# RWKV attention with two MLPs on one core: the first units rearranged

## Chip, core and metric

The kernel runs on one core of a Trainium2 chip. The metric is the device time of one execution, in microseconds (us). TensorE multiplies, VectorE (DVE), ScalarE (ACT) and GpSimd (POOL) do the rest, and SyncE (SP) issues the DMA transfers.

## What is computed

Everything is float32. Attention with a decaying state over 4 batches, 8 heads, 768 steps, head size 48; its output goes through two MLPs for 3072 tokens of width 384.

```python
state = zeros(B, H, D, D)                      # 4, 8, 48, 48
for t in range(768):
    cur = einsum('bhd,bhe->bhde', u[None] * k[t], v[t])
    y[t] = einsum('bhd,bhde->bhe', r[t], state + cur)
    state = w[t][..., None] * state + einsum('bhd,bhe->bhde', k[t], v[t])
x = y as [3072, 384]
h = x @ w_in                                   # 384 x 1024
solu = h * softmax(h)
x = layernorm(solu) * g_ln @ w_out             # 1024 x 384
g = relu(x @ w2_in) ** 2                       # 384 x 2048
out = g @ w2_out                               # 2048 x 384
```

## The kernel before

The 768 steps are cut into NU = 12 units of T = 64 steps. Within a unit the decay products are built by doubling: `w_products` makes six levels of products of w, and at each of the 6 levels `carry` (VectorE) multiplies halves of r and `carry_k` (GpSimd) halves of k by them, `right_halves` (ScalarE) copies r into a layout for TensorE, `level` (TensorE) multiplies k with r and `pair_scores` (VectorE) takes the wanted scores out of PSUM into `att`. `place` and `take_level5` (ScalarE) finish the scores. Each step is done for two halves (h = 0, 1) of the heads. At level 0 stands `level_bonus`: k with r of odd steps, and the product `uk` = k times u with r. That product is made on GpSimd (`products`), which also decays the state (`decay_state`) and clears the score tile.

Then come `k_natural` (transposes of k in TensorE, copied by `take_k` into the same buffer `uk`), `output` (state and scores times r and v; two copies `take_output` take it to `x_t`) and `state_step` with `add_state`. `repack` is six small DMA transfers that move heads into rows; `x_high` and `x_low` split x into two parts, since float32 products are made of three products of such parts.

PSUM has 8 banks: `flex` has four (banks 0 and 1 for attention, 2 and 3 for the first MLP), `hid` one and `acc` three for the second MLP. The first MLP runs one unit behind the attention: `hidden1` for two token tiles t of 128 tokens and two column halves f, `row_max`, `exps`, `gate`, `squares`, `variance`, `inverse_root`, `normalise`, then `ln_transpose` with `ln_high` and `ln_low`, and `narrow1` for three row tiles d with `take_narrow`. The second MLP works on blocks of two units, from turn 3 on: `up` into `hid`, `relu`, `square`, `down` into `acc`, sixteen times a block.

One turn handles one unit of attention. In each turn every engine has its own written order: the tables SP_AT, PE_AT, DVE_AT, ACT_AT and POOL_AT give each step a place in the queue of its engine (a number for each half, tile or piece). Turns 0, 1 and 2 have tables of their own, as have turns 3 and 4; from turn 5 on two tables alternate. Engines work their queue strictly in order and wait for each other with semaphores. Steps placed alongside the attention in turns 0 to 4 are the weights' pieces: 24 pieces are loaded (`load_piece`), and split by ScalarE (`piece_high`) and VectorE (`piece_low`); the second MLP's are also stored to DRAM (`keep_piece`) and reloaded later (`load_w2`).

Before the first turn SyncE issues, in this order, k, r_pair (two), u, w, r and gain of unit 0, then weight pieces and v. VectorE, ScalarE and GpSimd wait with `wait_ge(u_loaded, 32)` for both u and gain before any turn. In `state_step` TensorE waits for `x_ready` since it writes the banks from which the output is copied; the next `level_bonus` waits for `state_ready`, the end of the add, for the same reason; and `k_natural` waits for `att_ready`, since the transposes go over the last scores in banks 0 and 1. `output` waits for `knat_ready`. Half 0 of `hidden1` for t = 1 waits for `solu_ready`, as both token tiles use banks 2 and 3. ScalarE's activations all show line 888, its common helper.

## Time and profile before

| | us |
|---|---|
| median of 3 runs | 826.29 |
| lowest and highest | 823.72, 828.02 |
| the profiled execution | 825.71 |
| its span, first to last instruction | 824.1 |
| TensorE busy in the span | 768.9 |
| VectorE, ScalarE, GpSimd busy | 493.6, 416.5, 200.0 |

The mean granted TensorE clock is 0.992 of full speed. How to read the rows: a time at the left is the start from the span's beginning, in us, then the duration; `x32` is a count of merged instructions; `[2.22 <-DVE state L703]` says that the engine had been idle for 2.22 us before and that this instruction released it. PEld is the weight load of TensorE, PE the matmul. L511 is line 511 of the kernel.

### The profile page before, as it was taken

The numbers are of one execution on the slowest core, as the hardware profiler recorded it, in microseconds if no ns is written. First come the engines' busy times: TensorE is split into PE (matmuls) and PEld (weight loads), VectorE is DVE, ScalarE is ACT, GpSimd is POOL, SyncE is SP. The second block draws the span as 40 slices with busy tenths as digits, with TensorE's granted clock in tenths as the row PEclk, the third lists the DMA queues.
The fourth block names the chain that finished last, engine by engine and source line by source line (L and its number), as shares of the span: only waits on it lengthen the run. The fifth ranks groups of instructions, "written<-read, shape, count | busy, mean of one in ns | idle before, by whom it ended". The sixth has DMA issues, their size and how long they took to land.

```text
span 824.1 us, 25081 instructions
## 1 busy us (share of the span) xinstructions
PE 768.9 (93%) x10480; PEld 642.2 (78%) x10480; DVE 493.6 (60%) x985; ACT 416.5 (51%) x853; POOL 200.0 (24%) x277
## 2 busy tenths in 40 slices
PE   1567879999999999999999999999999999999997
PEld 1456768788788788788788788788789788888886
DVE  7787576867856745736754746853755763453333
ACT  3855474845744643644653644553654562333232
POOL 5453334212413301412400501510501210000000
PEclk9989999999999999999999999999999999999999
DMA  7423454174375344535455444344544232453652
GB/s 237 122 86 80 164 163 133 63 244 176 117 243 160 112 173 164 168 104 165 130 180 158 138 141 166 131 149 147 179 141 147 98 118 82 153 163 121 227 192 102
DMA packets 32272, 122.34 MB, mean 148 GB/s; under 512 B 4896, under 2 KB 10144, under 8 KB 32160
## 3 DMA queue, kind: packets, MB, share of 16 engines
q1 hardware_dynamic: 32160, 120.74, 44.3%
q8 instruction: 83, 1.36, 0.7%
q14 instruction: 29, 0.24, 0.1%
HBM read 102.24 MB, written 17.30 MB: 145 GB/s over the span
## 4 chain that ended last, share of the span: by engine, by line
PE 87%; DVE 4%; ACT 3%; issue 2%; DMA 2%; SPq 1%; POOL 0%; DVEq 0%; POOLq 0%; ACTq 0%
PE hid L558 24%; PE acc L571 24%; PE flex L511 13%; PE flex L542 11%; PE flex L449 4%; PE flex L525 2%; PE flex L475 2%; PE flex L464 1%; PE flex L482 1%; PE flex L493 1%; PE flex L435 1%; DVE r_t L689 1%; DMA gain<-in_gcol 1%; DVE w_up L675 1%; PE flex L430 1%
## 5 line engine op out<-in xcount | busy, mean ns | idle before, releaser
L558 PE MATMUL hid<-y_hi,w 128*128 128x512 f32 x576 | 198.0, 398 | 0.1
L571 PE MATMUL acc<-g_hi,w 128*128 128x512 f32 x576 | 195.7, 396 | 1.4 <-DVE g_lo L766 0.9
L888 ACT ACTIVATE r_right<-r_t 64x256 f32<-64x256 f32 x240 | 100.2, 417 | 69.2 <-DVE r_t L689 53.8
L762 DVE TENSOR_TENSOR act<-act 128x512 f32<-128x512 f32 x96 | 68.9, 718 | 105.0 <-ACT g_hi L888 105.0
L571 PEld LDWEIGHTS acc<-g_hi,w 128*128 128x128 f32 x576 | 108.1, 188 | 25.2 <-issue 1.2
L558 PEld LDWEIGHTS hid<-y_hi,w 128*128 128x128 f32 x576 | 108.1, 188 | 23.8 <-issue 0.5
L888 ACT ACTIVATE act<-hid 128x512 f32<-128x512 f32 x96 | 57.3, 597 | 118.5 <-PE hid L558 118.1
L1098 POOL TENSOR_TENSOR k_t<-k_t,w_up 128x256 f32<-128x256 f32 x120 | 86.0, 733 | 113.8 <-PE flex L449 85.0
L558 PE MATMUL hid<-y_lo,w 128*128 128x512 f32 x288 | 112.5, 391 | 0.0
L571 PE MATMUL acc<-g_lo,w 128*128 128x512 f32 x288 | 112.4, 390 | 0.0
L542 PE MATMUL flex<-ln_hi,out_hi 128*128 128x256 f32 x288 | 81.1, 282 | 1.6 <-issue 0.8
L542 PE MATMUL flex<-ln_hi,out_lo 128*128 128x256 f32 x288 | 80.8, 281 | 0.0
L542 PE MATMUL flex<-ln_lo,out_hi 128*128 128x256 f32 x288 | 80.8, 281 | 0.0
L766 DVE TENSOR_TENSOR g_lo<-act,g_hi 128x512 fp32r<-128x512 f32 x96 | 68.3, 712 | 3.3
L689 DVE TENSOR_TENSOR r_t<-r_t,w_up 128x256 f32<-128x256 f32 x120 | 66.3, 568 | 6.3 <-ACT r_right L888 5.7
L449 PEld LDWEIGHTS flex<-r_right,k_t 128*32 128x32 f32 x3072 | 34.6, 116 | 40.7 <-issue 28.6
L888 ACT ACTIVATE g_hi<-act 128x512 fp32r<-128x512 f32 x96 | 60.7, 632 | 6.1 <-PE acc L571 3.3
L449 PE MATMUL flex<-r_right,k_t 128*32 128x32 f32 x3072 | 41.2, 205 | 23.2 <-DVE att L665 13.7
L511 PE MATMUL flex<-in_hi,x_hi 128*128 128x512 f32 x144 | 61.2, 425 | 1.0 <-DVE x_lo L708 0.7
L571 PEld LDWEIGHTS acc<-g_lo,w 128*128 128x128 f32 x288 | 54.2, 188 | 10.0
L558 PEld LDWEIGHTS hid<-y_lo,w 128*128 128x128 f32 x288 | 54.2, 188 | 10.0
L511 PE MATMUL flex<-in_hi,x_lo 128*128 128x512 f32 x144 | 58.3, 405 | 0.0
(92 smaller groups left out, 1199.6 us busy)
## 6 DMA issues: line engine op xcount, KB each, us to landing
w<-split_w SPq DMA_DIRECT2D x80, 768.0 KB, 4.6
split_w<-w SPq DMA_DIRECT2D x16, 768.0 KB, 5.9
k_t<-in_kT SPq DMA_DIRECT2D x12, 512.0 KB, 3.9
r_pair<-in_rT SPq DMA_DIRECT2D x24, 256.0 KB, 4.3
w_t<-in_wT SPq DMA_DIRECT2D x12, 512.0 KB, 6.0
r_t<-in_rT SPq DMA_DIRECT2D x12, 512.0 KB, 6.5
v_n<-in_vN SPq DMA_DIRECT2D x12, 384.0 KB, 5.4
out<-o_stage SPq DMA_DIRECT2D x5, 768.0 KB, 7.3
```

The costliest lines, as they stand in the source:

```text
L449: last = mm(flex[block_rows(q % 2 * 2 + n), h, c:c + BK], k_t[:, o:o + BK], right[:, :, o // 2:(o + BK) // 2], start=True, stop=True)
L475: mm(flex[half_rows(i), b2, x * T:(x + 1) * T], state[u % 2][:, q, i], r_t[:, q * T:(q + 1) * T], start=x == 0, stop=False, skip_group_che ...
L511: last = mm(flex[:, MLP1 + f, :], x[:, k, toks], w[:, k, cols], start=n == 0, stop=n == len(terms) - 1)
L525: last = nc.tensor.transpose(flex[:, MLP1 + half, n * P:(n + 1) * P], solu[:, t, j * P:(j + 1) * P], ident[:, :])
L542: last = mm(flex[:, MLP1 + d % 2, 0:TOK], w[:, j, rows], x[:, j, :], start=n == 0, stop=n == len(terms) - 1)
L558: last = mm(hid[:, :], w2[:, j % RING, w, k * P:(k + 1) * P], y[:, k, :], start=n == 0, stop=n == len(terms) - 1)
L571: last = mm(acc[:, d], w2[:, j % RING, w, rows], gx[:, j % 2], start=j == 0 and n == 0, stop=j == J2 - 1 and n == 2, skip_group_check=True)
L689: e.tensor_tensor(right, right, left_w, ALU.mult).then_inc(r_ready, 1)
L762: e.tensor_tensor(act[:, j % 2], act[:, j % 2], act[:, j % 2], ALU.mult).then_inc(g_ready, 1)
L766: e.tensor_tensor(g_lo[:, j % 2], act[:, j % 2], g_hi[:, j % 2].bitcast(F32), ALU.subtract).then_inc(glo_ready, 1)
L888: return nc.scalar.activation(out_, in_, func, **more)
L1098: e.tensor_tensor(left, left, right_w, ALU.mult).then_inc(k_ready, 1)
```

## The change

- On the zero state of unit 0 nothing is done any more: no `decay_state` in turn 0; `add_state` of unit 0 copies instead of adding.
- `products` moves from GpSimd to ScalarE: for each half two activations of 128x256 with u as a scale per row.
- Unit 0 is loaded in halves with semaphores of their own (`r_first` and so on, `wait_loaded`); ScalarE issues the two halves of w, then u between them, then gain. gain has its own semaphore, awaited at the first piece of the output weights.
- In units 0, 1 and 2 (`FILL = 3`) the transposes of k and the state step go to banks of the second MLP, idle until then (`side_bank`: `hid` and the last of `acc`). There `k_natural` waits for the state of the unit before and not for the scores, `state_step` waits for the copies of k and not for the output's, and the next `level_bonus` waits for the output's copies and not for the state.
- In the first MLP's units 0 and 1 the second token tile goes to `acc[:, 0:2]` (`h_banks`), and its `hidden1` doesn't wait for the first tile's gate; nor do the transposes wait for it.
- `output` waits for `att_ready`, and for `knat_ready` only from unit 3 on.
- All tables of order are written anew. In turns 1 and 2 `hidden1` of the first token tile stands ahead of level 1, and in turn 1 the first half of the second tile between the halves of level 1; in turn 3 `hidden1` comes first. SyncE issues v ahead of the repack in turns 1, 3 and 4.

```diff
 SP_AT = [
-    {"load_w_pair": 1, "load_k": 3, "repack": 6, "load_r": 5, "load_v": 9, "load": {5: 0, 6: 2, 7: 4, 9: 7, 8: 8}},
-    {"load_w_pair": 1, "load_k": 0, "repack": 2, "load_r": 4, "load_v": 7, "keep": {9: 6, 8: 8}, "load": {11: 3, 10: 5}},
+    {"load_w_pair": 1, "load_k": 5, "repack": 6, "load_r": 4, "load_v": 8, "load": {5: 0, 7: 2, 6: 3, 8: 7, 9: 9}},
+    {"load_w_pair": 1, "load_k": 2, "repack": 4, "load_r": 5, "load_v": 3, "keep": {8: 6, 9: 8}, "load": {10: 0, 11: 7}},
...
 PE_AT = [
-    {"level": ((0, 1), (2, 3), (4, 5), (6, 7), (8, 9), (10, 11)), "k_natural": 12, "output": 13, "state": 14},
-    {"level": ((0, 1), (4, 5), (6, 7), (8, 10), (11, 12), (14, 15)), "k_natural": 16, "output": 18, "state": 20, "hidden1": ((2, 3), (9, 13)), "ln":
-     (17, 19), "narrow": (21, 22, 23)},
-    {"level": ((0, 1), (2, 5), (6, 7), (8, 9), (11, 12), (14, 15)), "k_natural": 16, "output": 18, "state": 20, "hidden1": ((3, 4), (10, 13)), "ln":
-     (17, 19), "narrow": (21, 22, 23)},
+    {"level": ((0, 1), (2, 3), (4, 5), (6, 7), (8, 9), (10, 11)), "k_natural": 12, "output": 13, "state": 14, "read_state": -1},
+    {"level": ((0, 1), (4, 6), (7, 8), (9, 10), (11, 13), (14, 16)), "k_natural": 17, "output": 18, "state": 20, "hidden1": ((2, 3), (5, 12)), "ln":
+     (15, 19), "narrow": (21, 22, 23)},
+    {"level": ((0, 1), (4, 5), (6, 7), (8, 9), (11, 12), (14, 15)), "k_natural": 17, "output": 18, "state": 20, "hidden1": ((2, 3), (10, 13)), "ln":
+     (16, 19), "narrow": (21, 22, 23)},
...
 ACT_AT = [
-    {"right": ((1, 4), (6, 8), (9, 10), (11, 13), (14, 17)), "place": (15, 16), "level5": (18, 19), "k_natural": 20, "output": 22, "x_high": 24,
-     "piece": {0: 0, 1: 2, 2: 3, 3: 5, 4: 7, 5: 12, 6: 21, 7: 23}},
+    {"products": (1, 2), "right": ((0, 3), (5, 7), (9, 11), (13, 14), (16, 18)), "place": (15, 17), "level5": (19, 20), "k_natural": 24, "output": 22,
+     "x_high": 26, "piece": {0: 4, 1: 6, 2: 8, 3: 10, 4: 12, 5: 21, 6: 23, 7: 25}},
+    {"products": (0, 2), "right": ((1, 3), (5, 6), (8, 9), (12, 13), (14, 16)), "place": (15, 17), "level5": (19, 20), "k_natural": 23, "output": 24,
+     "x_high": 27, "exp": (7, 18), "squares": (11, 21), "ln_high": (22, 25), "narrow": (26, 28, 29), "piece": {8: 4, 9: 10}},
...
+        def wait_loaded(eng, first, rest, u, h, each=16):
+
+            if u or h:
+                eng.wait_ge(rest, each * (u + 1))
+            else:
+                eng.wait_ge(first, each)
+
...
+        def side_bank(u, n):
+
+            if u >= FILL:
+                return flex[:, n]
+            return acc[:, KD - 1] if n else hid[:, :]
+
+        def h_banks(u, t):
+
+            return acc[:, 0:2] if t and u < FILL - 1 else flex[:, MLP1:MLP1 + 2]
...
-            load_k(0)
-            load_w_pair(0)
-            sp.dma_start(u_rows[:, :], uT).then_inc(u_loaded, 16)
-            sp.dma_start(w_t[:, :], wT[0]).then_inc(w_in, 16)
-            load_r(0)
-            sp.dma_start(gain[:, :], gcol).then_inc(u_loaded, 16)
+            for h in range(2):
+                sp.dma_start(k_t[:, half(h)], kT[0][:, half(h)]).then_inc(k_in if h else k_first, 16)
+                for i in range(2):
+                    sp.dma_start(r_pair[half_rows(i), i, half(h)], rT[0][half_rows(i), half(h)])                        .then_inc(rp_in if h else rp_first, 16)
+                sp.dma_start(r_t[:, half(h)], rT[0][:, half(h)]).then_inc(r_in if h else r_first, 16)
...
+                wait_loaded(pe, k_first, k_in, u, h)
+                wait_loaded(pe, rp_first, rp_in, u, h, 32)
                 if h == 0:
-                    pe.wait_ge(k_in, (u + 1) * 16)
-                    pe.wait_ge(rp_in, (u + 1) * 32)
-                    wait(pe, state_ready, u * 2)
+                    wait(pe, x_ready if u <= FILL else state_ready, u * 2)
...
                     pe.wait_ge(k_ready, half_count(u, LEVELS - 1, h))
-                    pe.wait_ge(att_ready, u * 2 + h + 1)
+                    if u < FILL:
+                        wait(pe, state_ready, u * 2)
+                    else:
+                        pe.wait_ge(att_ready, u * 2 + h + 1)
...
-                pe.wait_ge(knat_ready, (u + 1) * 2)
+                pe.wait_ge(att_ready, (u + 1) * 2)
+                if u >= FILL:
+                    pe.wait_ge(knat_ready, (u + 1) * 2)
...
-                pe.wait_ge(x_ready, u * 2 + 2)
+                if u < FILL:
+                    pe.wait_ge(knat_ready, u * 2 + 2)
+                else:
+                    pe.wait_ge(x_ready, u * 2 + 2)
...
-                elif f == 0:
+                elif f == 0 and u >= FILL - 1:
                     pe.wait_ge(solu_ready, u * 2 + 1)
...
-            v.wait_ge(u_loaded, 32)
...
+            def products(u, h):
+                wait_loaded(s, k_first, k_in, u, h)
+                wait(s, state_mm, u)
+                for p in range(h * NP // 2, (h + 1) * NP // 2):
+                    cols = slice(p * TOK, (p + 1) * TOK)
+                    last = a(uk[:, cols], k_t[:, cols], ACT.Copy, scale=u_rows[:, p:p + 1])
+                last.then_inc(uk_ready, 1)
...
+            for h in range(2):
+                s.dma_start(w_t[:, half(h)], wT[0][:, half(h)]).then_inc(w_in if h else w_first, 16)
+                if h == 0:
+                    s.dma_start(u_rows[:, :], uT).then_inc(u_loaded, 16)
+            s.dma_start(gain[:, :], gcol).then_inc(gain_loaded, 16)
...
-            s.wait_ge(u_loaded, 32)
+            s.wait_ge(u_loaded, 16)
...
-                if i == at["decay"] and u < NU - 1:
+                if i == at["decay"] and 0 < u < NU - 1:
                     decay_state(u)
```

## Rows read from the trace of the kernel before

**Rows 1.** The page: busy us (share) and count by engine; TensorE in 40 slices.
```profile
PE 768.9 (93%) x10480; PEld 642.2 (78%) x10480; DVE 493.6 (60%) x985; ACT 416.5 (51%) x853; POOL 200.0 (24%) x277
...
PE   1567879999999999999999999999999999999997
```
**Rows 2.** Stretches cut where units begin: length, busy us by engine, PEclk, DMA share, GB/s.
```profile
0.00:44.47 44.47, 15.83 (x552) 12.86 (x553) 32.34 (x55) 26.26 (x50) 21.47 (x37) 1.00 0.59 178
44.47:90.03 45.56, 35.03 (x741) 29.51 (x741) 32.43 (x71) 24.30 (x53) 16.46 (x22) 0.89 0.33 89
90.03:130.50 40.47, 32.03 (x747) 27.52 (x750) 26.65 (x56) 23.83 (x53) 16.85 (x22) 0.96 0.42 140
130.50:824.10 693.60, 685.98 (x8449) 572.30 (x8448) 402.15 (x805) 342.07 (x697) 145.17 (x196) 1.00 0.45 151
```
**Rows 3.** TensorE's waits, 0 to 200 us: us in total, times, longest.
```profile
PE flex L449 <- DVE att L665: 13.7, 7, 6.4
PE flex L430 <- DMA r_pair<-in_rT: 8.4, 1, 8.4
```
**Rows 4.** Two stretches of turn 0.
```profile
0.00:8.43 8.43, 0.00 (x1) 0.03 (x2) 5.29 (x11) 4.99 (x3) 2.64 (x17) 1.00 0.82 182
...
21.03:34.58 13.55, 6.55 (x288) 5.06 (x289) 10.73 (x23) 12.93 (x32) 6.89 (x10) 1.00 0.39 107
```
**Rows 5.** Timeline of turn 0, start to last score copy: start, us, instruction, idle before.
```profile
11.04 2.48 POOL L1080 TENSOR_TENSOR uk<-k_t,u_rows 128x512 f32<-128x512 f32 x2 [7.23 <-DMA gain<-in_gcol]
...
16.04 3.73 POOL L1107 TENSOR_TENSOR state<-state,w_up 64x768 f32<-64x768 f32 x2 [0.34 <-DVE w_up L675]
16.75 3.31 DVE L689 TENSOR_TENSOR r_t<-r_t,w_t 128x256 f32<-128x256 f32 x2
18.48 0.87 ACT L888 ACTIVATE r_right<-r_t 64x256 f32<-64x256 f32 x2 [5.75 <-DVE r_t L689]
...
33.33 2.24 ACT L888 ACTIVATE att<-flex 32x128 f32<-32x128 f32 x8
```
**Rows 6.** Groups of instructions: count, busy us, mean ns of one, idle before.
```profile
L689 DVE TENSOR_TENSOR r_t<-r_t,w_up 128x256 f32<-128x256 f32 x120 | 66.3, 568 | 6.3 <-ACT r_right L888 5.7
...
L888 ACT ACTIVATE y_new<-flex 128x256 f32<-128x256 f32 x36 | 13.8, 382 | 75.9 <-PE flex L542 75.8
...
L888 ACT ACTIVATE out_hi<-act,gain 128x384 fp32r<-128x384 f32 x2 | 1.1, 608 | 0.0
```
**Rows 7.** Timeline from the output of unit 0 to the first hidden matmul.
```profile
37.53 1.96 PE L482 MATMUL flex<-att,v_n 64*48 64x64 f32 x64 [0.73 <-issue]
...
44.47 0.66 PE L430 MATMUL flex<-r_pair,k_t 128*32 128x32 f32 x32 [2.22 <-DVE state L703]
...
45.82 0.84 ACT L888 ACTIVATE x_hi<-x_t 128x768 fp32r<-128x768 f32 x1 [2.94 <-DMA x_t<-x_t]
...
48.00 0.47 PE L511 MATMUL flex<-in_hi,x_hi 128*128 128x512 f32 x1 [0.73 <-DVE x_lo L708]
```
**Rows 8.** TensorE's timeline where it waits, turns 1 and 2.
```profile
54.32 1.42 PE L449 MATMUL flex<-r_right,k_t 128*32 128x32 f32 x64 [1.87 <-DVE att L665]
56.42 0.66 PE L449 MATMUL flex<-r_right,k_t 128*32 128x32 f32 x32 [0.69 <-DVE att L665]
...
70.42 0.63 PE L464 MATMUL flex<-ident,k_t 128*128 128x128 f32 x4 [1.09 <-ACT att L888]
72.64 0.63 PE L464 MATMUL flex<-ident,k_t 128*128 128x128 f32 x4 [1.59 <-ACT att L888]
...
94.34 0.46 PE L449 MATMUL flex<-r_right,k_t 128*32 128x32 f32 x32 [2.62 <-DVE att L665]
```
**Rows 9.** Chain of work, two merged pieces (start, us); and one stretch with its clock.
```profile
60.47 4.14 PE flex L511 x9
...
66.44 2.30 PE flex L511 x9
...
54.32:60.14 5.82, 2.97 (x154) 2.52 (x154) 5.67 (x17) 4.10 (x8) 3.06 (x5) 0.51 0.01 3
```

219 lines of the change are left out of this document (113 added, 106 removed).

## Prediction

> **What bounds the kernel now.** Read the shares of the page first, then the forty slices, then stretches cut where a unit begins. TensorE is busy nearly everywhere and thin only in the first five slices [rows 1]. Cut at the first matmul of units 1, 2 and 3 (44.47, 90.03, 130.50), the table of stretches says how much is to be had: TensorE is idle 44.47 - 15.83 = 28.6 us in turn 0, 10.5 in turn 1, 8.4 in turn 2, and only 693.6 - 686.0 = 7.6 in all that follows [rows 2]. The change neither adds nor removes a matmul (the state terms of unit 0 are already skipped), so what comes after 130.5 us costs the same and starts earlier: the prediction is how much earlier unit 3 starts. A second loss is the granted clock: 0.89 over turn 1 and 0.96 over turn 2 [rows 2].
>
> Next comes who TensorE waits for: the first loads (8.4) and above all the scores on VectorE (13.7) [rows 3]. Inside turn 0, from 21.0 to 34.6 us, ScalarE works 12.93 of 13.55 us: there it is the bound, not TensorE with 6.55 [rows 4].
>
> **Turn 0, the start.** Before, GpSimd's product stands until 11.04, released by the small load of gain, and then GpSimd decays the zero state for 3.73 us from 16.04 while VectorE's first carry waits for w and runs for 1.66 us a half (3.31 for two) beside it [rows 5]; such a carry has a mean of 0.57 us elsewhere [rows 6]. First ScalarE copy of r: 18.48 [rows 5]. After, gain gates nothing before the output weights, the decay is gone, and the first carry stands ahead of the w products. Its operands are first halves. k, r_pair, r and w halves are 1.05 MB; with w's other half moving along on the second issuing queue about 1.3 MB. Before, 182 GB/s x 8.43 us = 1.53 MB had arrived by 8.43 [rows 4], so 1.3 MB is there by 7.2; I take 7.8 for its landing. Bounds: 7.3 (VectorE's set-up, estimated from its 5.29 us of work that begins at 1.3) and 11.0 (as late as gain was). With a carry of 0.7 ScalarE's first copy is at 8.6.
>
> The Trainium skill speaks against that step: "DMA: Bandwidth & Descriptors", section Issuing engines are not separate DMA queues, says that loads issued from several engines share the same 16 DMA engines and interleave, so that only issuing time is saved. It is weighed as a rival below.
>
> **Turn 0, the ScalarE chain.** From 18.48 to the end of the last score copy at 33.33 + 2.24 = 35.57, ScalarE works nearly without a gap: 17.1 us [rows 5]. Into that stretch come the products, four activations of 128x256 a unit with a scale taken per row. Bounds: 0.38 us (plain, 128x256) and 0.61 us (128x384 with the gain column) [rows 6]; nearer the first by size, plus a little for the column: 0.48, so 1.9 us. Weight piece 0 comes in too (it used to lie in idle time; 0.84, as x_hi of the same shape [rows 7]) and piece 5 goes out behind (2 x 0.61) [rows 6]. Chain: 17.1 + 1.9 + 0.8 - 1.2 = 18.6, and 1.0 for waits that its tighter start opens: 8.6 + 19.6 = 28.2.
> By "ScalarE: Activation LUTs" of the Trainium skill, section What ACT_TABLE_LOAD costs, a plain activation is 186 ns + 0.833 ns an element and a column operand adds about 93 ns: an estimate of 0.49 us a product, 2.0 a unit, which would leave the sum as it is.
>
> The output matmuls now need only the scores; the transposes of k and their two copies went ahead of them before, and begin at 37.53 [rows 7]. After: 28.4, which is 9.1 earlier.
>
> **Turn 0 to the first hidden matmul.** Before, 10.5 us lie between the output (37.53) and hidden (48.00): output 2.0, copy, six repack DMAs, x_hi at 45.82, x_lo [rows 7]. The same 10.5 after gives 38.9. But ScalarE is in order: the products of unit 1 stand behind x_high, which waits for the repack, and their second half stands behind the first copy of r, which waits for VectorE's carry behind x_low. x_hi is done 45.82 + 0.84 - 9.1 = 37.5, first product half 38.5; x_low and carry to 39.4, copy of r (2 x 0.42) 40.3, second half 41.3, its 32 matmuls 42.4. This is a new wait that takes part of the gain: hidden starts at 42.4, 5.6 earlier. Level 1 of unit 1 waited 1.87 us more for scores at 54.32 [rows 8]; VectorE's chain is 8 to 9 earlier, so now TensorE itself is last: 42.4 + 4.3 for two hidden tiles = 46.7, **7.6 earlier**. The state step with its add (wait of 2.2 at 44.47 [rows 7]) lies inside the wait for the repack.
>
> **Turn 1.** From 54.32 on. (a) Hidden tile t=1, first half, needs no gate of t=0 any more, since it goes to an idle bank; it stands between the halves of level 1, where the gaps were (0.69 at 56.42 is the next [rows 8]; they are most of the 13.7 of [rows 3]), and fills them with a little less than its 2.30 us [rows 9]: 2.1. (b) The k transposes waited 1.09 and 1.59 for score copies [rows 8]; in an idle bank they wait only for k, and the output needs the copies still: 2.0 of 2.7. (c) The same nine hidden matmuls took 4.14 us at 60.47 and 2.30 at 66.44 [rows 9]: the first in or near a stretch with a granted clock of 0.51, that is 1.2 and not 2.4 GHz, in which TensorE worked 2.97 of 5.82 us [rows 9]. If the gaps are filled this 1.8 goes; I count half, 0.9. Together **5.0**. Both ends: 0 (VectorE or ScalarE is the bound) and 10.5 + 5.0 (all idle time, and 11% of 45.6 us of clock).
>
> **Turn 2.** The wait of 2.62 at 94.34 (r had landed late) [rows 8] gets both hidden tiles in front: 2.6. The k transposes again: the pair waits are the same kind, 2.7, of which 2.5. New: the products of unit 2 stand behind ScalarE's copy of the last narrow tile, and GpSimd had them done ahead; 0.38 + 0.97 + two handings over, less 0.4 of k matmuls: 1.1 of wait. Net **4.0**; both ends -1.1 and 8.4 + 1.6.
>
> **Unit 3 on.** Hidden now comes first in turn 3, right behind the last narrow tile whose copy it needs: 0.6 lost. GpSimd loses 2.1 us a unit and ScalarE gains 1.9, nine times; it is at half load [rows 1], the product has from the state step to the next unit to run, and down or hidden matmuls (2.3 each) stand between the last narrow tile and the scores that want it: nothing. If that cover is gone it costs 1.9 a unit. The order of all the other turns is dealt out anew; with 7.6 us idle there [rows 2] it can win 2 at most and lose as much or more; zero.
>
> **Sum.** 7.6 + 5.0 + 4.0 - 0.6 = 16.0. Profiled execution 825.71 (span 824.1): 809.7; the median of the runs is 0.6 above that execution: **810.3**.
>
> **The rivals.**
> *Loads don't come early* (the rule named above): halves interleave, and the first complete only as the whole does, near 10.97. Mechanism here: DMA already moves 182 GB/s in that stretch. Everything in turn 0 is 3.2 later, in full: 813.5. For it: bandwidth, not issue, bounds the loads. Against: the halves are half the bytes. 15%.
> *The small engines take the place.* VectorE and ScalarE are busy 32.4 and 24.3 of 45.6 us in turn 1 [rows 2], in chains of halves that hand over to each other; if TensorE's gaps are theirs, turns 1 and 2 give only 1: 825.7 - 7.6 - 1 + 0.6 = 818. 17%.
> *All gaps close*: turn 0 as above, turns 1 and 2 lose three quarters of the 19 idle and 6.6 clock microseconds less what level 1 took already: 7.6 + 17 = 24.6: 801. 15%.
> *The new order gives it back*: waits of some 1.6 us in each of nine steady turns: 14.4, and the time stays at 824.7. 5%.
> *Slower: products in front of relu.* ScalarE's queue is strict, and relu frees the only hid bank. If the product waits there for k or for the state step with a relu behind it, TensorE stops for that wait. At 1.8 us a unit in nine units the 16 are gone; at 3 it is 27: 837. Against: GpSimd's product was over long before the next unit's scores. 4%.
> The forecast itself has the remaining 44%, with a range of its own of 804 to 815.
>
> **How the numbers follow.** 0.5% is 4.1 us, about what a measurement of this kernel can tell from no change. Faster by more: 44 + 15 + 17 + 15 = 91%; within: 5; slower: 4. The range reaches over the small-engine case and most of the case in which all gaps close: 799 to 822.
>
> **What would show it.** After: output matmuls of unit 0 at about 28, first hidden at 42, unit 2 near 77, unit 3 near 114; a product of 0.48 us; the second half of unit 1's u matmuls released by ScalarE; no wait of the k transposes for score copies; the rest from unit 3 on 693 to 695 us. It is wrong if ScalarE's chain in turn 0 is not the bound any more (then the output comes before 26), if turn 1 keeps its gaps, or if the rest grows.

## The result, and the profile after

The changed kernel has a median of 832.11 us over 20 runs, the kernel before 823.72 us over 20 beside it. The ratio is **1.0088 (95% interval 1.0070 to 1.0107)**: slower by 0.9%, where 1.9% faster was forecast and the range ended at 822. The profiled execution took 832.73 us, its span 831.0 us, 6.9 more than before.

The page of the changed kernel, busy time by engine and the first slices, answers [rows 1].

```profile
PE 775.3 (93%) x10480; PEld 647.2 (78%) x10480; DVE 485.5 (58%) x991; ACT 434.0 (52%) x901; POOL 168.5 (20%) x251
...
PE   3478878999999999999999999999999999999997
...
PEclk9878899999999999999999999999999999999999
```

TensorE issues the same 10480 matmuls and is busy 6.4 us longer with them; its idle time is 55.7 us against 55.2. The first two slices fill sooner (34 against 15), the sixth and seventh are no fuller (78 against 79), and PEclk is under 9 in four of the first six.

The changed kernel cut where units 1 and 2 begin, at turn 3's first matmul (now a hidden one; it starts at 129.89, the cut is 0.2 us later), and where units 5 and 11 begin; columns as in [rows 2].

```profile
0.00:39.70 39.70, 14.99 (x552) 12.53 (x553) 26.08 (x55) 27.55 (x54) 13.68 (x31) 0.96 0.66 200
39.70:86.48 46.78, 37.27 (x741) 31.16 (x741) 29.71 (x69) 26.05 (x57) 14.53 (x20) 0.82 0.33 97
86.48:130.05 43.57, 34.91 (x742) 29.72 (x742) 28.52 (x64) 26.20 (x59) 13.99 (x20) 0.88 0.32 98
130.05:264.21 134.16, 130.86 (x1777) 108.00 (x1776) 93.90 (x180) 81.95 (x168) 29.39 (x40) 0.99 0.52 177
264.21:648.16 383.95, 379.69 (x5306) 317.78 (x5305) 225.10 (x476) 203.55 (x435) 85.27 (x120) 1.00 0.44 146
648.16:831.00 182.84, 177.56 (x1368) 147.97 (x1367) 82.14 (x152) 68.67 (x129) 11.66 (x20) 1.00 0.41 140
```

The same stretches of the kernel before from unit 3 on, not shown so far:

```profile
130.43:260.40 129.97, 129.38 (x1778) 107.27 (x1777) 94.18 (x181) 77.78 (x157) 35.41 (x44) 1.00 0.51 168
260.40:640.24 379.84, 378.93 (x5306) 317.16 (x5305) 226.75 (x476) 195.28 (x411) 97.85 (x132) 1.00 0.46 151
```

Against [rows 2], the first three turns have 42.9 us of idle time on TensorE (24.7, 9.5, 8.7) and not 47.6: 4.7 saved. Its busy time there is 87.2 us and not 82.9: 4.3 given back, for the same matmuls. Turn 3 therefore begins at 130.05 and not 130.50, where 114 was forecast. Turns 3 and 4 then take 4.3 more (134.16 against 129.9), turns 5 to 10 take 4.1 more (idle 4.3 against 0.9), and the rest 1.0 less. Sum: -0.45 + 4.3 + 4.1 - 1.0 = 6.9.

**Turn 0.** The timeline of the changed kernel where [rows 5] and the first line of [rows 7] stood.

```profile
7.92 0.65 PE L446 MATMUL flex<-r_pair,k_t 128*32 128x32 f32 x32 [7.92 <-DMA r_pair<-in_rT]
8.78 0.42 DVE L716 TENSOR_TENSOR r_t<-r_t,w_t 128x256 f32<-128x256 f32 x1 [1.48 <-DMA r_t<-in_rT]
...
9.31 0.88 ACT L925 ACTIVATE r_right<-r_t 64x256 f32<-64x256 f32 x2 [1.62 <-DVE r_t L716]
...
24.90 0.78 PE L465 MATMUL flex<-r_right,k_t 128*32 128x32 f32 x38 [2.86 <-issue]
...
29.09 2.23 ACT L925 ACTIVATE att<-flex 32x128 f32<-32x128 f32 x8
...
32.07 1.41 PE L503 MATMUL flex<-att,v_n 64*48 64x64 f32 x64
```

The chain on ScalarE starts 9.2 us sooner (9.31 against 18.48) and ends only 4.2 sooner (31.3 against 35.6). In its middle TensorE pauses for 2.86 us with nothing recorded to wait for ("issue"), until 24.90, and the other three engines stand behind it (ScalarE 3.58, VectorE 3.71, GpSimd 3.37 us). Behind the output, the state step waits 2.70 us (at 36.18) for the copies of k, which the new table of ScalarE puts behind a copy of the output and pieces of weights.

**Into turn 1.** The same kernel from the first matmul of unit 1 to its k transposes, where [rows 7, 8] stood.

```profile
39.70 0.66 PE L446 MATMUL flex<-r_pair,k_t 128*32 128x32 f32 x32 [1.55 <-DMA k_t<-in_kT]
40.78 0.84 ACT L925 ACTIVATE x_hi<-x_t 128x768 fp32r<-128x768 f32 x1 [3.65 <-DMA x_t<-x_t]
...
42.48 1.08 PE L451 MATMUL flex<-r_pair,uk 128*32 128x64 f32 x32 [2.12 <-ACT uk L925]
42.99 0.91 ACT L925 ACTIVATE r_right<-r_t 64x256 f32<-64x256 f32 x2 [0.56 <-DVE r_t L716]
...
44.89 1.08 PE L451 MATMUL flex<-r_pair,uk 128*32 128x64 f32 x32 [0.91 <-ACT uk L925]
45.90 0.80 PE L535 MATMUL flex<-in_hi,x_hi 128*128 128x512 f32 x1
46.49 0.63 PE L535 MATMUL flex<-in_lo,x_hi 128*128 128x512 f32 x1
...
52.07 0.46 PE L465 MATMUL flex<-r_right,k_t 128*32 128x32 f32 x32
...
66.70 1.84 PE L549 MATMUL flex<-ident,solu 128*128 128x128 f32 x8 [2.01 <-DVE solu L778]
...
70.54 0.66 PE L483 MATMUL acc<-ident,k_t 128*128 128x128 f32 x4 [0.37 <-POOL k_t L1144]
```

ScalarE waits 3.65 us for the repack, and the products behind x_hi make TensorE wait 2.12 and 0.91. The eighteen hidden matmuls take from 45.90 to 52.07, 6.2 us, against 4.4 before (48.00 to 52.45): the first nine take 0.55 to 0.80 us each, mostly 0.63, the others 0.40. The k transposes wait 0.37, not 1.09 and 1.59; a new wait of 2.01 for solu stands before the transposes of the first MLP, which the new order puts ahead of the second half of level 5.

**Unit 3's loads.** The same kernel, SyncE's queue and who is late behind it.

```profile
120.51 4.49 SPq L332 DMA_DIRECT2D x_t<-x_t  x6
125.04 0.58 SPq L325 DMA_DIRECT2D v_n<-in_vN  x1
125.78 1.14 SPq L312 DMA_DIRECT2D r_pair<-in_rT  x2
126.98 0.57 SPq L313 DMA_DIRECT2D w_t<-in_wT  x1
...
133.57 2.11 POOL L1144 TENSOR_TENSOR k_t<-k_t,w_t 128x256 f32<-128x256 f32 x2 [15.07 <-DMA w_t<-in_wT]
...
140.78 0.46 PE L465 MATMUL flex<-r_right,k_t 128*32 128x32 f32 x32 [2.42 <-DVE att L691]
```

The new table of turn 2 puts `load_w_pair` at 5, behind load_k, repack and load_v. SyncE issues r_pair and w of unit 3 at 125.78 and 126.98 (before: 110.62 and 112.54). GpSimd waits 15.07 us for w, and TensorE 2.42 at its level matmuls. In turn 2 itself, TensorE has a second long pause without a recorded wait, 2.14 us up to 116.75, in the middle of the output matmuls.

### The profile page after: what moved, and what is told of

Its sections match the earlier page's. It is cut to its first block, busy times and chain, and to the rows that moved or that the text cites. A ratio compares the mean times of both kernels' runs of the same rounds, so it can differ in the third digit from the quotient of the medians.

```text
span 831.0 us, 25138 instructions
## 1 busy us (share of the span) xinstructions
PE 775.3 (93%) x10480; PEld 647.2 (78%) x10480; DVE 485.5 (58%) x991; ACT 434.0 (52%) x901; POOL 168.5 (20%) x251
## 4 chain that ended last, share of the span: by engine, by line
PE 86%; DVE 4%; issue 3%; DMA 2%; SPq 2%; ACT 2%; POOL 0%; DVEq 0%; POOLq 0%; ACTq 0%
PE acc L597 24%; PE hid L584 24%; PE flex L535 11%; PE flex L566 10%; PE flex L465 4%; PE flex L496 3%; PE flex L549 2%; PE flex L503 2%; PE acc L535 2%; SPq L332 1%; DMA r_t<-in_rT 1%; PE flex L451 1%; PE flex L517 1%; DVE r_t L716 1%; PE flex L483 1%
## 5 line engine op out<-in xcount | busy, mean ns | idle before, releaser
L1144 POOL TENSOR_TENSOR k_t<-k_t,w_t 128x256 f32<-128x256 f32 x24 | 20.8, 886 | 239.9 <-PE flex L451 211.6
L716 DVE TENSOR_TENSOR r_t<-r_t,w_up 128x256 f32<-128x256 f32 x120 | 60.2, 523 | 5.6 <-ACT r_right L925 5.5
L691 DVE COPY_PREDICATED att<-mask,flex 128x128 f32<-128x128 uint32 x120 | 41.3, 355 | 37.0 <-PE flex L465 36.1
L465 PE MATMUL flex<-r_right,k_t 128*32 128x32 f32 x3072 | 42.4, 205 | 19.4 <-DVE att L691 6.9
```

Of the source, the lines that this page charges most:

```text
L465: last = mm(flex[block_rows(q % 2 * 2 + n), h, c:c + BK], k_t[:, o:o + BK], right[:, :, o // 2:(o + BK) // 2], start=True, stop=True)
L691: e.copy_predicated(dst, keep, src).then_inc(level_taken, 1)
L716: e.tensor_tensor(right, right, left_w, ALU.mult).then_inc(r_ready, 1)
L1144: e.tensor_tensor(left, left, right_w, ALU.mult).then_inc(k_ready, 1)
```

## The experiments

"Parts" are all changes of the kernel but the new tables of order; a ratio is to the kernel before, with its 95% interval. Fillers are extra matmuls whose result nothing reads.

### Order or parts: four kernels

**e1**, the parts with the tables of before; the products stand first in ScalarE's queue of each turn:

```diff
 # all tables as in the kernel before, except
-POOL_AT: "products": (0, 1)
+ACT_AT: "products": (0, 1), every other place + 2
```


> The changed kernel with the order tables of the kernel before; only the products stand first in ScalarE's turn, and are gone from GpSimd's. Theory A (the new order of the turns is what costs; the new parts by themselves gain as predicted): 0.980 to 0.990 of before, with turn 2 near 38 us and the rest from unit 3 on as before. Rival B (the parts themselves cost, through ScalarE's products and a granted clock that is low for longer): 1.003 to 1.010, granted clock under 0.985. Rival C (both give half): 0.995 to 1.000.

Measured: 822.29 us against 824.79, ratio 0.9964 (0.9942 to 0.9985). The gain is smaller than theory A had it; by the number it is rival C. The parts gain, and the new order takes more than they give: 1.0088 - 0.9964 = 0.0124.

**e2**, e1 with the new tables from turn 3 on. **e3**, the changed kernel with e1's tables from turn 3 on:

```diff
 # e2: turns 0 to 2 of all five tables as e1, the others as the changed kernel
 # e3: turns 0 to 2 as the changed kernel, the others as e1
```


> The changed kernel with the old order in turns 0 to 2 and the new one from turn 3 on. Theory A: if the loss lies in the first turns' order (w and r_pair of unit 3 issued at 125.8 us, behind everything), this is 0.985 to 0.993; the new order later costs the 3 us of waits that the trace shows from turn 3 on. Rival B: 1.00 to 1.01, as the changed kernel.

> The changed kernel with the new order in turns 0 to 2 and the old one from turn 3 on. Theory A: only the waits after turn 3 go, about 3 to 4 us of the 8: 1.003 to 1.006. Rival (the loss is all after turn 3): 0.998 or less. Rival B: no change against the changed kernel, 1.009.

Measured: e2 824.16 us, 0.9981 (0.9960 to 1.0002); e3 828.48 us, 1.0036 (1.0014 to 1.0058). e3 came out as expected, e2 between its two theories. The split between early and late turns depends on the way that one goes. By e3, the new order of turns 0 to 2 costs 1.0036 - 0.9964 = 0.0072, and that of the later turns 1.0088 - 1.0036 = 0.0052. By e2, the later turns cost 0.9981 - 0.9964 = 0.0017 and the first three 1.0088 - 0.9981 = 0.0107. Both ways the first three turns are the larger part. The stretch of turns 5 to 10, first e2, then e3:

```profile
255.74:641.79 386.05, 381.12 (x5305) 319.00 (x5305) 225.14 (x476) 203.60 (x435) 85.32 (x120) 1.00 0.43 146
```
```profile
266.93:647.38 380.45, 379.14 (x5306) 317.27 (x5305) 228.04 (x476) 204.83 (x435) 85.94 (x120) 1.00 0.45 151
```

With the new tables (changed kernel and e2) this stretch is 384 to 386 us and TensorE idle 4.3 to 4.9; with the old (before, e1 and e3) 380 to 381 and idle 1.3 or less. In the waits of TensorE from 264 to 648 us in the changed kernel all of the 4.1 us is put down to "issue", time in which it waits for nothing recorded; more on that below.

**e5**, the kernel before with nothing but the product moved:

```diff
-            def products(u, h):   # GpSimd, one operation a half
-                e.tensor_tensor(uk[:, half(h)]..., k_t[:, half(h)]..., u_rows..., ALU.mult)
+            def products(u, h):   # ScalarE, first in its queue of each turn
+                for p in range(h * NP // 2, (h + 1) * NP // 2):
+                    last = a(uk[:, cols], k_t[:, cols], ACT.Copy, scale=u_rows[:, p:p + 1])
```


> The kernel before with one part alone: k times u on ScalarE, first in its turn, everything else old. Theory A: near nothing, 0.999 to 1.003 (a wait of about 1 us in turns 1 and 2, none later). Rival B (ScalarE's products stall TensorE in every unit): 1.005 to 1.01, some 0.5 to 1 us of wait before the u matmuls in each of twelve units.

Measured: 825.86 us, 1.0006 (0.9984 to 1.0028). Unit 1 begins at 41.26, 3.2 sooner, and unit 3 at 124.39, 6 sooner; turns 3 and 4 give 4.9 of it back (134.9 against 130.0). In the trace of e1 one sees where: its windows and the timeline at the start of turn 3.

```profile
123.43:259.20 135.77, 131.56 (x1778) 108.58 (x1778) 93.41 (x181) 82.35 (x169) 30.80 (x40) 0.99 0.50 161
```
```profile
42.66 1.08 PE L419 MATMUL flex<-r_pair,uk 128*32 128x64 f32 x32 [5.92 <-ACT uk L893]
...
123.53 0.38 ACT L893 ACTIVATE y_new<-flex 128x256 f32<-128x256 f32 x1 [1.60 <-PE flex L534]
123.95 1.67 ACT L893 ACTIVATE y_hi<-y_new 128x512 fp32r<-128x512 f32 x3
125.52 1.69 ACT L893 ACTIVATE uk<-k_t,u_rows 128x256 f32<-128x256 f32 x4
126.47 0.65 PE L419 MATMUL flex<-r_pair,uk 128*32 128x64 f32 x32 [2.58 <-ACT uk L893]
```

ScalarE works in order, so the product comes behind the last narrow tile and the split of y (turn 3), behind the last narrow tile alone (turn 4, a wait of 0.87 us at 190.79), or behind x_hi and the repack (turn 1, 5.92 us). A product of 0.4 us costs TensorE 2.58 us in turn 3, and the clock falls a little as well (0.99). The other traces agree: turns 3 and 4 take 133.1 to 135.8 us in the three kernels with the old order there and the product on ScalarE (e1, e3, e5), and 129.9 to 130.5 in the eight with the old order and the product on GpSimd (before, e7, e7b, e8, e9, e10, e12, e17).

### The product's place and unit 3's loads

**e7** is e1, and **e4** the changed kernel, with the product back on GpSimd. **e6** is the changed kernel with `load_w_pair` ahead of `load_k` in turn 2. **e11** has both repairs.

```diff
 # e4 (from the changed kernel), e7 (from e1)
-ACT_AT: "products": ...
+POOL_AT: "products": (0, 1)
 # e6, SP_AT of turn 2; e11 is e4 + e6
-{"load_w_pair": 5, "load_k": 0, "repack": 3, "load_r": 2, "load_v": 4, ...
+{"load_w_pair": 0, "load_k": 1, "repack": 4, "load_r": 3, "load_v": 5, ...
```


> All new parts (halved first loads, no zero state, idle banks, second token tile) with the whole old order and k times u back on GpSimd. Theory D (the product on ScalarE is what takes the gain: behind x_high in turn 1, 5.9 us of wait in the run with the old order, and behind the narrow copies and y_high at the start of turns 3 and 4, 3.4 us of wait and 2 us of clock): 0.986 to 0.991, no wait of the u matmuls on the product in turns 3 and 4, turns 3 and 4 together 130 us as before instead of 135.8. Rival (the later turns lengthen whenever unit 3 starts early, because the weights of the second MLP aren't there): turns 3 and 4 still near 135 us and 0.996.

> The changed kernel with its new order, k times u back on GpSimd alone. Theory D: the waits of 2.1, 0.9 and 0.9 us on the product in turns 1 and 2 go: 2 to 4 us less than the changed kernel, 1.003 to 1.006. If the order of the turns is the larger part, still over 1.003; if the product is all, under 1.000.

> The changed kernel with one place moved: in turn 2 SyncE issues w and r_pair of unit 3 first, not after the repack and v (125.8 us in the trace). Theory E (late loads of unit 3 cost): w lands before 115, the carry of unit 3 isn't held to 133.9, the wait of 2.4 us for scores at 140.8 goes and some of the low clock behind it: 2 to 4 us less, 1.004 to 1.006. Rival: TensorE's other work hides it, 1.009 as the changed kernel.

> The changed kernel with two repairs at once: unit 3's w and r_pair issued first in turn 2, and k times u on GpSimd. If the two repairs add up (0.0059 and 0.0029 off 1.0088): 0.998 to 1.002. What is left above 0.9932 is then the rest of the new order. If they repair the same wait: 1.002 to 1.005.

| | us | before | ratio | interval |
|---|---|---|---|---|
| e7 | 818.85 | 824.35 | 0.9932 | 0.9904 to 0.9959 |
| e4 | 829.16 | 824.35 | 1.0059 | 1.0028 to 1.0091 |
| e6 | 828.94 | 824.35 | 1.0029 | 0.9997 to 1.0062 |
| e11 | 827.46 | 825.14 | 1.0013 | 0.9988 to 1.0038 |

e4 and e11 came out as expected, e7 gained less than theory D had it, though turns 3 and 4 did go back to 130 us, and e6 gained more than theory E. The product on ScalarE costs 0.0032 in the old order (e1 less e7) and 0.0029 in the new (changed kernel less e4). Each is within the intervals alone; that two orders give the same size speaks for it, and so do the turns 3 and 4 above. In the new order the place is another: the waits for the product in turn 1 (2.12 and 0.91 us) are a single one of 0.46 in e4. One line of SyncE's table costs 0.0059 (changed kernel less e6) or 0.0046 (e4 less e11), the largest single term found; for the first pair the intervals don't meet. Both repairs together give 0.0075, nearly their sum of 0.0088. Queue, windows and the once late level matmul of e6:

```profile
89.79 1.15 SPq L280 DMA_DIRECT2D r_pair<-in_rT  x2
90.98 0.59 SPq L281 DMA_DIRECT2D w_t<-in_wT  x1
...
134.73 0.46 PE L433 MATMUL flex<-r_right,k_t 128*32 128x32 f32 x32 [1.01 <-DVE att L659]
```
```profile
85.72:127.65 41.93, 33.71 (x750) 28.54 (x749) 30.04 (x66) 28.09 (x64) 14.32 (x20) 1.00 0.42 139
127.65:257.11 129.46, 127.27 (x1769) 105.64 (x1769) 91.81 (x178) 79.75 (x164) 29.87 (x40) 1.00 0.50 169
```

The loads leave 36 us earlier, and the wait for scores is 1.01 and not 2.42. These two rows are cut at the first matmul of unit 3, behind nine hidden ones. On the cut used above for the changed kernel, turn 3 of e6 begins at 125.38, and turns 3 and 4 take 131.7 us against 134.3; in e11 and e4 it is 131.4 against 135.3. So 2.6 and 3.9 us of the gain lie in turns 3 and 4. e6's turn 2 is shorter too, by 3.8 us, with a clock of 1.00; e11's is not, so that part may be chance. The late loads cost most in e3: its TensorE stands still for 4.26 us up to 133.81, at the first matmul of unit 3, whose r_pair was issued at 126.84 and takes some 5 us to land. The profile calls this wait "issue"; that it is the load is inferred from these times.

The windows of e7's first turns show what the parts are worth by themselves, and the one matmul line where most of it is lost again.

```profile
37.21:82.81 45.60, 33.65 (x740) 28.53 (x740) 35.12 (x78) 25.32 (x55) 19.02 (x24) 0.89 0.37 104
82.81:123.80 40.99, 33.28 (x741) 28.20 (x740) 26.39 (x58) 23.70 (x53) 16.73 (x22) 0.92 0.42 140
123.80:253.78 129.98, 129.39 (x1779) 107.28 (x1778) 94.55 (x181) 77.77 (x157) 35.39 (x44) 1.00 0.52 168
```
```profile
45.14 0.77 PE L503 MATMUL flex<-in_hi,x_hi 128*128 128x512 f32 x1 [4.18 <-DVE x_lo L712]
```

Turn 0 ends 7.3 us sooner (37.21 against 44.47). Turns 1 and 2 are 86.6 us, against 86.0 before: no part of the forecast 9 us comes here, even in the old order (the same program gave 91.0 in e7b, and 83.2 with other matmuls ahead of it in e17). TensorE now waits 4.18 us for x_lo where it waited 0.73 [rows 7].

### Which of the parts

**e8** is e7 without the idle banks, **e9** e7 with them in unit 0 alone.

```diff
-FILL = 3
+FILL = 0    # e8
+FILL = 1    # e9
```


> As the run with GpSimd's products and the old order, but without the idle banks: k transposes, state step and second token tile back in banks 0 to 3. What is left of the change is the halved first loads and gain's own semaphore and no decay of the zero state. If the idle banks gain what I predicted for them (the k transposes' waits of 2.7 us in turns 1 and 2), this is 3 to 5 us slower than that run; if the chain behind is VectorE's and ScalarE's, the two agree within 1.5 us and this is 0.988 to 0.993.

> The run with all parts, the old order and GpSimd's products, but FILL = 1: k transposes and state step of unit 0 alone go to idle banks; units 1 and 2 and the second token tile as in the kernel before. Theory F (the idle banks help turn 0 by 2 to 3 us, where nothing else is to be done, and cost 2 to 3 us in each of turns 1 and 2, with more time at the low clock): unit 3 starts near 119.5 us and this is 0.988 to 0.992, the fastest of all. Rival (the two runs with and without banks differ by chance): unit 3 near 122 to 124, 0.993 to 0.995.

Measured: e8 821.57 us against 824.35, 0.9947 (0.9913 to 0.9982); e9 819.30 against 825.14, 0.9918 (0.9897 to 0.9939). Half loads and the zero state alone thus carry 0.0053 of e7's 0.0068. e8 falls between its two expectations; e9 has the ratio of theory F but the start of unit 3 of its rival. That the banks gain anything in turns 1 and 2 is not to be seen (e9 with one unit of them is at 0.9918, e7 with three at 0.9932). Whether they cost anything there stays open: unit 3 begins at 123.26 in e9, 123.80 in e7, and in e8, whose turn 0 is 3 us longer, already at 121.69, but e8's profile was its fastest run (817.32, median 821.57).

### Gaps in which TensorE waits for nothing

The gaps that the trace puts down to issue sum to 10.2 us in the changed kernel and 5.1 in the kernel before. From 130 us on they are 4.4 us in the changed kernel, 5.1 in e2, 3.5 to 4.2 in e4, e6 and e11, and 0.6 to 2.3 with the old order there (before, e1, e5, e7 to e10, e12, e7b; and e3 without its wait of 4.26 us for a load, 1.2). Before 130 us they are 5.8 in the changed kernel, 3.3 to 5.0 in e4, e6, e11 and e3, 2.9 before, and 0 to 2.2 in the other kernels named so far. They often cut a group of like matmuls in two. Two of the changed kernel's:

```profile
317.84 0.39 PE L566 MATMUL flex<-ln_hi,out_hi 128*128 128x256 f32 x1 [1.24 <-issue]
...
398.70 0.45 PE L465 MATMUL flex<-r_right,k_t 128*32 128x32 f32 x29 [1.39 <-issue]
```

To see whether they belong to the order or to the place in TensorE's stream of instructions, the stream is shifted: **e14**, **e15**, **e16** are the changed kernel, **e17** is e7, with 24, 48, 96 and 48 short matmuls in the time before the first loads.

```diff
             pe.wait_ge(init_p, 2)
+            for n in range(24):   # 48, 96; 48
+                mm(hid[0:32, 0:32], ident[:, 0:32], ident[:, 0:32], start=True, stop=True)
             pe.wait_ge(init_v, 4)
```


> The changed kernel with 24 small matmuls (32 columns, into an idle bank) ahead of everything, in the time in which TensorE waits for the first loads. Across the runs so far TensorE's gaps with nothing recorded to wait for (issue) sum to 10.1 us in the changed kernel and 5.1 in the kernel before; kernels with the new later tables have 3.4 to 4.8 us of them in turns 5 to 10, those with the old tables 0 to 2.1. Theory A, stream position: these gaps are a late supply of instructions, and depend on where in TensorE's stream a dense run of short matmuls meets it; a shift of the whole stream moves them to other instructions, and their sum in turns 5 to 10 comes out otherwise than 4.1 (0.5 to 3, or over 5.5), the time with it. Theory B, order: they belong to the order of the work itself; 3.4 to 4.8 us at the same instructions (317.84 and 398.70 in the changed kernel), ratio 1.009 as without.

> As the run with 24, with 48. Theory A: the gaps of turns 5 to 10 stand at yet other instructions and their sum differs from that with 24 by over 1 us. Theory B: the same instructions, 3.4 to 4.8 us, ratio 1.009.

> As the run with 24, with 96. Theory A: sum differs again by over 1 us from at least one of the others; the ratios of the three shifts spread over more than 0.003. Theory B: the same instructions, 3.4 to 4.8 us, ratio 1.009, all three within 0.002.

> The parts with the old order and the product on GpSimd, with the same 48 small matmuls ahead. Without them the issue gaps summed to 2.1 and 3.2 us over the span in two profiles, ratio 0.9932 and 0.9949. Theory A: the low sum was the luck of its stream position; with a shift it may rise to 5 to 10 us, ratio 0.997 to 1.003. Theory B: it stays at 1 to 4 us, ratio 0.991 to 0.996.

| | us | before | ratio | interval | gaps, 260 to 645 | gaps from 130 on |
|---|---|---|---|---|---|---|
| changed kernel | 832.11 | 823.72 | 1.0088 | 1.0070 to 1.0107 | 4.1 | 4.4 |
| e14 | 830.27 | 824.59 | 1.0066 | 1.0027 to 1.0106 | 0.7 | 4.5 |
| e15 | 829.61 | 824.59 | 1.0057 | 1.0021 to 1.0093 | 1.8 | 4.2 |
| e16 | 829.01 | 824.59 | 1.0046 | 1.0015 to 1.0078 | 0.7 | 6.0 |
| e17 | 818.92 | 824.59 | 0.9936 | 0.9908 to 0.9964 | 1.5 | 1.5 |

The 48 and 96 matmuls also run over: the first real matmul is at 8.91 in e15 and at 12.27 in e16, not at 7.92. The gaps moved: none of the two above is left in any of the three. In their place stand others, in e14, e15 and e16:

```profile
197.37 0.32 PE L465 MATMUL flex<-r_right,k_t 128*32 128x32 f32 x3 [3.80 <-issue]
```
```profile
242.94 0.68 PE L517 MATMUL flex<-v_n,uk 64*64 64x48 f32 x32 [2.04 <-issue]
...
523.86 0.32 PE L465 MATMUL flex<-r_right,k_t 128*32 128x32 f32 x11 [1.34 <-issue]
```
```profile
243.82 0.50 PE L584 MATMUL hid<-y_hi,w 128*128 128x512 f32 x1 [2.71 <-issue]
```

So where a gap stands follows the position in the stream (the first theory), and so does the sum of turns 5 to 10: 0.7, 1.8 and 0.7 us, and these turns take 379.8 to 381.6 us in the three shifts, as with the old order. But the gaps came back in turns 3 and 4, and the sum from 130 us on stays at 4.2 to 6.0 us with the new order and at 1.5 with the old (nearer the second theory). Ahead of 130 us, e17 has 4.2 us of gaps, so 5.7 in all, which is what the first theory said; its time did not follow (0.9936). The ratios of the three shifts lie within 0.0020, as the second expected, and all below the unshifted one, within the intervals.

The kept traces tell what TensorE waits for. Section 3 of the page has a DMA queue for instructions:

```profile
q8 instruction: 83, 1.36, 0.7%
```

These are 83 packets of 16 KB in the changed kernel, 84 with 24 or 48 matmuls more and 85 with 96: the number follows TensorE's stream. In all 19 traces together there are 86 gaps over 0.25 us put down to issue, and 80 of them end 1.2 to 1.6 us after the end of such a packet, although the packets start 7.8 us apart in the median and never closer than 3.2. Examples: 24.90 behind a packet of 22.40 to 23.42, 317.84 behind 315.47 to 316.45, 398.70 behind 396.30 to 397.24, and 197.37 in e14 behind 195.05 to 195.99. So in these gaps TensorE waits for its next instructions, as far as times can show it. Of the six others, four stand at the first matmul of unit 3 in kernels that load its r_pair late (e3, e4, e15, e16), and two at the output of unit 0 (before, e5). No run shows why a packet comes late, nor why the new order meets this more often.

### Is the clock the reason?

**e10** fills the gaps of e7 in turns 1 and 2 with matmuls; **e12** puts them into one wait; **e7b** is e7 once more, beside e12.

```diff
 # e10, behind each half of levels 1 to 4
+                                if u in (1, 2) and l < IN_BK:
+                                    for n in range(4):
+                                        mm(hid[:, 0:P], ident[:, :], ident[:, :], start=True, stop=True)
 # e12, ahead of the first hidden matmul of unit 0
+                        for n in range(7):
+                            mm(acc[:, 0, 0:P], ident[:, :], ident[:, :], start=True, stop=True)
```


> All parts, old order, GpSimd's products (0.9932 before), with four matmuls of 128x128 into an idle bank behind each half of levels 1 to 4 in turns 1 and 2, whose result is never read: 16 times about 0.5 us more of TensorE work, part of it inside waits. Theory G (the low granted clock, 10.0 and 6.6 us of low level in turns 1 and 2, is what lengthens them): the clock of turns 1 and 2 rises to 0.97 or more and they shorten by 1 to 4 us in spite of the fillers, 0.989 to 0.993. Rival H (the clock is a symptom; the chain over VectorE and ScalarE sets the length): turns 1 and 2 keep their length or grow by the 3 to 6 us of fillers, 0.993 to 1.000.

> All parts, old order, GpSimd's products, and seven matmuls of 128x128 into an idle bank in front of the first hidden matmul of unit 0, where TensorE waited 4.2 us for x_low; the result is never read. They take 1.9 us at the full clock and 3.9 at the low one, so they fit into the wait. Theory G (TensorE goes into turn 1 at the low level since it stood still, and pays for it in the hidden matmuls, 0.63 against 0.39 us each): those 18 matmuls take 4.4 us, not 6, the low time of turn 1 falls from 10 to under 6 us, and this is 1 to 3 us less than the run without. Rival H: the level doesn't depend on it or the chain behind takes the gain up: within 1 us of the run without.

> The same kernel without the seven matmuls, on the same chip, for the comparison: 0.9932 again, within 0.002.

Measured: e10 829.57 us against 825.14, 1.0051 (1.0026 to 1.0076); e12 817.08 against 824.11, 0.9912 (0.9884 to 0.9940); e7b 820.20 against the same, 0.9949 (0.9924 to 0.9973). e10 is slower than both its theories. Its fillers work 18.5 us; turns 1 and 2 are 9.9 longer than e7's, and PEclk of turn 1 is about as low as without them (0.90 against 0.89): no test of what a higher clock would bring. In e12 the expected first effect did not come: 13 of the first 18 hidden matmuls still take 0.63 us. Its median is 3.1 us below e7b's, but the intervals overlap. Inconclusive, both.

What did come out is how much one program differs from itself. The windows of turns 1 and 2 of e7b, the program of e7 above, on another chip, in what was its slowest run (824.09 us, median 820.20):

```profile
36.90:84.68 47.78, 36.42 (x740) 30.35 (x740) 34.03 (x77) 25.39 (x55) 18.82 (x24) 0.82 0.34 97
84.68:127.90 43.22, 34.16 (x742) 29.41 (x741) 26.27 (x58) 23.61 (x53) 16.39 (x22) 0.88 0.40 135
```

Unit 3 begins at 127.90 and not 123.80; TensorE is idle 20.4 us in the two turns and not 19.7, and busy 70.6 and not 66.9, with a granted clock of 0.82 and 0.88 and not 0.89 and 0.92. So a single trace says nothing of differences under some 4 us in these turns. Over all runs: the mean granted clock is 0.991 to 0.992 for the kernel before in each of five groups (127 runs) and 0.989 to 0.994 for the kernels with the old order in turns 0 to 2 (e1, e2, e5, e7 to e10, e7b, e12). It is 0.979 for the changed kernel and e3, 0.984 to 0.985 for e4, e6 and e11, and 0.968 to 0.973 for the shifted e14 to e16. Within the kernel before, runs under 0.9905 average 1.8 to 4.1 us more than the others, by group. But e17 has a mean clock of 0.978 and the time of e7 (0.9936 and 0.9932). Its low part stands in turn 0: from 15 to 30 us PEclk reads 0.50 in e17 and 1.00 in e7, and yet 32 matmuls of level 1 take 0.65 us at 16.18 in e17 and 0.66 at 16.70 in e7. So the mean clock misleads where turn 0 is in it, in e15 and e16 too (0.66 and 0.77 there).

In turns 1 and 2 alone, length and clock roughly go together (e10, with its fillers, left out). Twice one less the granted clock, times the length, gives the time at the lower level, one profile each:

| | low, us | turns 1 and 2, us |
|---|---|---|
| e5, e8 | 7 | 83.1, 81.4 |
| e12, e17, e9 | 10 | 84.9, 83.2, 86.9 |
| before | 14 | 86.0 |
| e7, e1, e2, e14 | 17 | 86.6, 87.2, 87.7, 88.0 |
| e6, e16 | 18 | 85.7, 84.3 |
| e4, e11, e15 | 24 | 86.9, 87.2, 88.2 |
| changed kernel, e7b | 27 | 90.2, 91.0 |
| e3 | 33 | 94.7 |

Which of the two makes the other is not shown. The new order of the first turns goes with more time at the lower level, and what part of its cost that is stays open.

## Why the prediction was wrong

**Measured and forecast, along the path.** The forecast of turn 0 and what follows went by six points.

| | before | forecast | after |
|---|---|---|---|
| ScalarE's first copy of r | 18.48 | 8.6 | 9.31 |
| end of the last score copy | 35.57 | 28.2 | 31.3 |
| output matmuls | 37.53 | 28.4 | 32.07 |
| x_hi starts | 45.82 | 36.7 | 40.78 |
| first hidden matmul | 48.00 | 42.4 | 45.90 |
| level 1 of unit 1 | 54.32 | 46.7 | 52.07 |

- **The start was right**, within 0.7 us, partly by luck: r and w landed for VectorE at 8.78 and not 7.8, but the carry took 0.42 us and not 0.7. The first matmul gained 0.5 (7.92 against 8.43), though its operands were half as large. The 9 us on ScalarE come from the decay and the product on GpSimd, from gain's gate and from the carry's place ahead of the w products. For the loads themselves the Trainium skill ("DMA: Bandwidth & Descriptors", section Issuing engines are not separate DMA queues) was nearer than the halves: transfers interleave, only issuing is saved. As a rival for the whole start it fell: nothing was 3.2 us later.
- **The chain's length was mis-sized**: 22.0 us and not 19.6. The product is 1.71 us for four, 2.0 by the group's mean of 497 ns, against 0.48 each forecast: right. The "1.0 for waits that its tighter start opens" was too small, and it was not ScalarE that failed: TensorE's one gap of 2.86 us at 24.90, a wait for instructions, is more than the whole difference of 2.4. The other profiles with the new order of turn 0 have it too (2.3 to 2.9 us in e3, e4, e6, e11, e15 and e16); e14 has 1.92 and 1.30 and a chain of 19.9. Against the old order the early start is worth nothing:

```profile
14.41 0.87 ACT L893 ACTIVATE r_right<-r_t 64x256 f32<-64x256 f32 x2 [1.52 <-DVE r_t L684]
```

  e1's chain begins 5.1 us later, takes 17.1 us as before, since its products came earlier, and ends at 31.48, where the changed kernel's ends too. e1's unit 1 begins at 36.28, the changed kernel's at 39.70.
- **x_hi and the products behind it**: the mechanism was right, and e1 shows it at 5.92 us in the plain old order.
- **Level 1 gained 2.3, not 7.6.** Of the 5.4 missing, 3.5 had been lost by the first hidden matmul, 3.1 of them by the end of the scores, and 1.9 went on the two hidden tiles at the lower clock level: 6.2 us, not the 4.3 taken from a stretch at the full one. These are the terms that failed in the sum: the chain, and hidden tiles priced at the full clock although the forecast made them the path's last piece. The clock alone would not have saved it: in e4 the 18 run at the full level (45.27 to 49.7), and level 1 then waits 1.89 us for scores and begins at 51.61.
- **Turn 1: -5.0 forecast.** From level 1 to unit 2's first matmul it is 34.4 against 35.7 us: -1.3. The parts (a) and (b) did what they say: the half tile stands between the halves of level 1 at 52.46, and the k transposes wait 0.37. But each wait was replaced: 2.01 for solu, 1.10 for k, 0.99 and 0.61 for r and scores. Part (c), the clock, went the other way: 0.82, not 0.89. One comparison proves little here (e7b), so take all: of the kernels with all the parts, cut at turn 3's first matmul, four have turns 1 and 2 together under the 86.0 us of before (e17 83.2, e16 84.3, e12 84.9, e6 85.7); the others, in either order, have 86.6 to 94.7, and e10 with its fillers 96.5. None is near the 77 forecast. The rival "the small engines take the place" (818, 17%) is nearest for the parts by its number: e7 measured 818.85, e1, with the product on ScalarE as in the forecast, 822.29. That VectorE and ScalarE hold these gaps open was not tested.
- **Turn 2: -4.0 forecast, +3.1 measured**, 2.9 of it more busy time at a granted clock of 0.88. The 2.62 of [rows 8] at level 1 did go, and so did the waits of the k transposes; 2.14 for instructions and 1.45 and 1.25 for scores came in their place.
- **"Dealt out anew ... zero" is the step that turned the sign.** The order costs 0.0124 to 0.0127, some 10 us (by the three shifted kernels, against e1, rather 7 to 8). I had read SyncE's table for turns 1, 3 and 4 (v ahead of the repack) and passed over turn 2, in which r_pair and w of unit 3 fall behind it; I priced a moved step at nothing without looking at who waits for it. This one line is 0.0059, 4.9 us. The rival "the new order gives it back" had 5% and gave it as waits in nine steady turns (14.4 us); there, TensorE has 3.4 us more idle time in six turns, put down to issue, and in the shifted kernels most of that is gone from these turns (idle 0.9 to 2.4).
- **The product off the critical path was wrong by its place**: "nothing" holds from turn 5 on (e1's turns 5 to 10 take 379.8 us, as before), but in the old order the product stands behind y_new and y_hi at the start of turn 3 and behind y_new at that of turn 4. The slower rival put the price in front of relu; no such wait is in the trace.

**Accounting.** New parts with the old order and the product on GpSimd: -0.0068 (e7). Product on ScalarE: +0.003. New order: +0.0125. The sum is +0.0087, measured +0.0088. Inside the new order, w_pair's place is 0.0046 to 0.0059, the later turns 0.0017 to 0.0052, and the rest of turns 0 to 2 lies between 0.001 and 0.006, by which pair one takes (each with an uncertainty of 0.003 or so). The forecast was a ratio of 0.981, so 0.028 is to be explained: 0.0125 the order priced at zero, 0.003 the product priced at nothing, and 0.0125 is missing from the parts, which gave 0.0068 where the forecast had 0.019. Open are three things: why turns 1 and 2 kept their length with the parts, why the instructions come late more often in the new order (2 to 4 us more from 130 us on, and 2.9 in turn 0), and whether a way to keep the clock up in turns 1 and 2 would pay.

**A better kernel.** The parts without the new order beat both: e12 at 0.9912, e9 at 0.9918 and e7 at 0.9932 (0.9949 in the second group) can't be told from each other, and the interval of each lies below one.

## What to carry to other kernels

Time gained in the fill of a pipeline is kept only if the next stage's own chain starts earlier too: follow the gain through the next two waits (here the repack, x_hi, x_lo) before it is booked. When an order is written anew, go through every queue, the DMA issuing one first, and ask of each load that moved back who waits for it; "zero" for a thousand small moves is a guess, and its downside is larger than its upside where the engine is 99% busy. An operation moved onto an in-order engine costs what stands ahead of it at the start of a turn, a DMA wait or another stage's copies, and not its own duration. And where an engine pauses with nothing recorded to wait for, look at the queue of instructions before the order is blamed.
